# Attention with a complex state and two expert mixtures: plain float32 products in place of three rounded ones

## What is computed

```python
# first mixture; N, D, E, F = 3072, 384, 8, 1024
do_compute = (x @ w_skip) > 0
e_idx = np.argmax(xc @ w_gate, axis=1)            # xc = x[do_compute]
for e in range(E):
    h = np.maximum(xc[mask] @ w1[e], 0.0)         # 384 -> 1024
    y[mask] = gate_w[mask, None] * (h @ w2[e])    # 1024 -> 384
out[do_compute] = xc + y
...
# second mixture: router on normalised rows, no skip, no residual
for e in range(E):
    h = np.maximum(x[mask] @ w1[e], 0.0)
    out[mask] = gate_w[mask, None] * (h @ w2[e])
```

## Time and profile before

| | before |
|---|---|
| median of three runs | 805.1 us |
| profiled execution: its time | 804.9 us |
| profiled execution: its span | 803.0 us |
| mean granted TensorE clock | 0.951 |
| PE, PE weight load busy | 700.5 us, 622.4 us |
| DVE, ACT busy | 657.8 us, 476.1 us |
| POOL busy | 212.9 us |
| first matmul of slot 0 | 372.87 us |
| start of the last matmul of slot 23 | 798.04 us |

### The profile page before, as it was taken

One profiled execution on the slowest core, in us unless ns is written; L12 is line 12 of the kernel. 1 busy time (PEld: TensorE's weight loads), 2 busy tenths in 40 slices (PEclk: granted clock), 3 DMA queues, 4 the chain that ended last, 5 costly groups with the idle time before them and its releaser, 6 DMA issues.

```text
span 803.0 us, 17480 instructions
## 1 busy us (share of the span) xinstructions
PE 700.5 (87%) x6568; PEld 622.4 (78%) x6568; DVE 657.8 (82%) x1241; ACT 476.1 (59%) x660; POOL 212.9 (27%) x184
## 2 busy tenths in 40 slices
PE   0577867169999999947999999999999999999997
PEld 0323332158888888847999998998999999999997
DVE  7998999989999999967888767756898696676672
ACT  7678988566676676552656544646544545544541
POOL 3000000031111111105153566532344322233422
PEclk9888989579999999977999999999999999999999
DMA  7463643017853332455666866776565755756630
GB/s 192 152 216 124 207 161 109 0 34 147 158 145 101 108 118 89 166 116 177 203 220 202 278 222 205 238 222 219 192 216 180 265 192 191 245 208 188 245 139 30
DMA packets 90900, 136.85 MB, mean 170 GB/s; under 512 B 22474, under 2 KB 70070, under 8 KB 90656
## 3 DMA queue, kind: packets, MB, share of 16 engines
q1 hardware_dynamic: 83680, 119.54, 47.9%
q0 software_dynamic: 7168, 16.64, 5.8%
HBM read 124.15 MB, written 14.01 MB: 172 GB/s over the span
## 4 chain that ended last, share of the span: by engine, by line
PE 47%; DVE 4%; DMA 2%; issue 1%; ACT 1%; POOL 0%; POOLq 0%; SPq 0%; DVEq 0%
PE banks L1385 23%; PE banks L1342 22%; PE banks L1328 2%; DVE mix_spot L1578 1%; DVE w_lo L972 1%; DMA raw<-w1b 1%; DMA mix_rows<-xbuf,lists 1%; DVE mix_hT_lo L1677 0%; DMA xbuf<-mix_y,to_scatter 0%; PE banks L1320 0%; ACT mix_hT_hi L1425 0%; DVE mix_y L1701 0%; ACT w_hi L961 0%; POOL to_scatter L1218 0%; POOLq L1091 0%
## 5 line engine op out<-in xcount | busy, mean ns | idle before, releaser
L1342 PE MATMUL banks<-mix_xT_hi,w_hi 128*128 128x240 f32 x576 | 158.8, 276 | 0.6 <-DVE mix_xT_lo L1686 0.6
L1342 PE MATMUL banks<-mix_xT_lo,w_hi 128*128 128x240 f32 x576 | 158.9, 276 | 0.0
L1342 PE MATMUL banks<-mix_xT_hi,w_lo 128*128 128x240 f32 x576 | 158.8, 276 | 0.0
L1385 PE MATMUL banks<-w_hi,mix_hT_hi 128*128 128x384 f32 (+3 forms) x384 | 135.7, 353 | 3.8 <-DVE mix_hT_lo L1677 3.8
L1385 PE MATMUL banks<-w_lo,mix_hT_hi 128*128 128x384 f32 (+3 forms) x384 | 129.8, 338 | 0.0
L1385 PE MATMUL banks<-w_hi,mix_hT_lo 128*128 128x384 f32 (+3 forms) x384 | 129.7, 338 | 0.0
L1425 ACT ACTIVATE mix_hT_hi<-banks 128x480 fp32r<-128x480 f32 x96 | 54.8, 572 | 111.0 <-PE banks L1342 106.0
L1342 PEld LDWEIGHTS banks<-mix_xT_hi,w_hi 128*128 128x128 f32 x576 | 109.5, 190 | 0.9 <-issue 0.8
L1342 PEld LDWEIGHTS banks<-mix_xT_hi,w_lo 128*128 128x128 f32 x576 | 109.6, 190 | 0.0
L1342 PEld LDWEIGHTS banks<-mix_xT_lo,w_hi 128*128 128x128 f32 x576 | 109.5, 190 | 0.0
L1677 DVE SCALAR_TENSOR_TENSOR mix_hT_lo<-banks,mix_hT_hi 128x480 fp32r<-128x480 f32 x96 | 62.7, 653 | 50.5 <-ACT mix_hT_hi L1425 50.4
(11 more groups left out here) (230 smaller groups left out, 1469.0 us busy)
## 6 DMA issues: line engine op xcount, KB each, us to landing
raw<-w1b SPq DMA_DIRECT2D x16, 1536.0 KB, 7.9
raw<-w2b SPq DMA_DIRECT2D x16, 1536.0 KB
A<-w2a_t SPq DMA_DIRECT2D x8, 1536.0 KB, 8.4
raw<-w1a SPq DMA_DIRECT2D x8, 1536.0 KB
raw<-w2a SPq DMA_DIRECT2D x8, 1536.0 KB
ring<-a SPq DMA_DIRECT2D x9, 864.0 KB, 5.1
qk<-q SPq DMA_DIRECT2D x48, 96.0 KB, 2.3
qk<-k SPq DMA_DIRECT2D x48, 96.0 KB, 2.3
```

The source lines that it names most:

```text
L1342: last = pe.matmul(pU[g % TURNS][:, n * N:(n + 1) * N], w1p[m][:, b, c, f * P:(f + 1) * P], xT[s][:, c, 0:N], start=(c == 0 and (s, m) == ...
L1385: last = pe.matmul(pD[0:m, half, 0:ph.width], hT[s][:, f, half * P:half * P + m], w2p[w][:, b, f, 0:ph.width], start=(f == 0 and (s, w) == ...
```

## The change

The mixtures' operands become plain float32 arrays, `xT`, `hT`, `w1` and `w2`, and each product is one `matmul` call on them. All splitting of weights, tokens and hidden numbers goes, on ACT and on DVE; ACT's ReLU (`hidden`) and its copy of the transposed tokens (`copy_x`) write the operands alone. Weights are loaded by DMA straight into the buffers that TensorE reads, two for each layer, by the parity of the slot. They are loaded two slots ahead: `load1(later)` once the first layer of this slot is done (`h_made`), `load2(later)` once its second layer is done (`y_made`). At the start, SP issues the second layer's weights of slot 0 and both layers' weights of slot 1 one after another. The semaphores for loads and scatters come in pairs, one for each parity. The transposes no longer wait for `y_ready`. ACT squares the results of the slot before (`square_y`) one step earlier, and DVE finishes both halves of the slot before ahead of everything else.

```diff
-        self.raw1 = raw1
-        self.raw2 = sbuf("raw2", [P, FC, DM + E])
-        self.hi1, self.lo1 = (sbuf(f"w1_{part}", [P, 2, KC, F], F32R) for part in ("hi", "lo"))
-        self.hi2, self.lo2 = (sbuf(f"w2_{part}", [P, 2, FC, DM + E], F32R) for part in ("hi", "lo"))
+        self.w1 = (raw1, sbuf("w1_odd", [P, KC, F]))
+        self.w2 = tuple(sbuf(f"w2_{b}", [P, FC, DM + E]) for b in range(2))
...
+    def load1(self, sp, slot, e):
+        w1 = slot.ph.weights[0][bass.ds(e, 1)].rearrange("e (c p) f -> p (e c) f", p=P)
+        sp.dma_start(self.w1[slot.b][:, :, :], w1).then_inc(slot.ph.loaded1[slot.b], 16)
...
-            weights.load(sp, Slot(phases[0], 0, 0, 0, 0), None, 0)
+            weights.load2(sp, Slot(phases[0], 0, 0, 0, 0), 0)
+            weights.load1(sp, Slot(phases[0], 0, 1, 1, 1), 1)
+            weights.load2(sp, Slot(phases[0], 0, 1, 1, 1), 1)
...
+                    sp.wait_ge(ph.h_made, slot.j * NG + NG)
+                    sp.sem_inc(weights.carrier, 1)
+                    weights.load1(sp, later, e)
...
+                if later is not None:
+                    sp.wait_ge(ph.y_made, slot.j * SUB + SUB)
+                    sp.sem_inc(weights.carrier, 1)
+                    weights.load2(sp, later, e)
...
-                pe.wait_ge(ph.lo1_ready, slot.j * 2 + 2)
-                pe.wait_ge(ph.x_lo, slot.j * SUB + SUB)
+                pe.wait_ge(ph.loaded1[b], slot.i * 16 + 16)
+                pe.wait_ge(ph.x_ready, slot.j * SUB + SUB)
...
-                            for s, m in PASSES:
-                                last = pe.matmul(pU[g % TURNS][:, n * N:(n + 1) * N],
-                                                 w1p[m][:, b, c, f * P:(f + 1) * P], xT[s][:, c, 0:N],
-                                                 start=(c == 0 and (s, m) == PASSES[0]),
-                                                 stop=(c == KC - 1 and (s, m) == PASSES[-1]))
+                            last = pe.matmul(pU[g % TURNS][:, n * N:(n + 1) * N],
+                                             weights.w1[b][:, c, f * P:(f + 1) * P], xT[:, c, 0:N],
+                                             start=(c == 0), stop=(c == KC - 1))
...
-                        for s, w in PASSES:
-                            last = pe.matmul(pD[0:m, half, 0:ph.width], hT[s][:, f, half * P:half * P + m],
-                                             w2p[w][:, b, f, 0:ph.width],
-                                             start=(f == 0 and (s, w) == PASSES[0]),
-                                             stop=(f == FC - 1 and (s, w) == PASSES[-1]))
+                        last = pe.matmul(pD[0:m, half, 0:ph.width], hT[:, f, half * P:half * P + m],
+                                         weights.w2[b][:, f, 0:ph.width], start=(f == 0), stop=(f == FC - 1))
...
                 hidden(slot, 0)
-                if nxt is not None and (ph.n, slot.at) != (0, 0):
-                    weights.hi_part1(act, nxt, 0)
-                hidden(slot, 1)
-                if nxt is not None and (ph.n, slot.at) != (0, 0):
-                    weights.hi_part1(act, nxt, 1)
```

More of the change, by code:

```diff
@@ L951, in part @@
[L951 to L974, removed]
@@ L984, with load2 @@
+    def load2(self, sp, slot, e):
+        ph, into = slot.ph, self.w2[slot.b]
+        w2 = ph.weights[1][bass.ds(e, 1)].rearrange("e (c p) f -> p (e c) f", p=P)
+        sp.dma_start(into[:, :, 0:w2.shape[2]], w2).then_inc(ph.loaded2[slot.b], 16)
+        if ph.scored:
+            sp.dma_start(into[:, :, w2.shape[2]:], ph.scoring[bass.ds(e, 1)].rearrange("e p c k -> p (e c) k")
+                         ).then_inc(ph.loaded2[slot.b], 16)
 class Phase:
@@ L1197, in body @@
                                  ).then_inc(routing_loaded, 16)
+                if later is not None:
+                    sp.wait_ge(ph.y_made, slot.j * SUB + SUB)
+                    sp.sem_inc(weights.carrier, 1)
+                    weights.load2(sp, later, e)
             tail, _ = stream(sp, phases, E, body)
             for ph in phases:
-                for s in range(SUB):
-                    sp.wait_ge(ph.scattered[s], tail.j * 16 + 16 if ph is tail.ph else 16 * E)
+                for done in ph.scattered[0] + ph.scattered[1]:
+                    sp.wait_ge(done, tail.i * 16 + 16 if ph is tail.ph else 8 * E)
                     sp.sem_inc(weights.carrier, 1)
@@ L1350, in body @@
                     pe.wait_ge(weighed, 2 if slot.at == 0 else 3)
-                pe.wait_ge(ph.lo2_ready, slot.j * 2 + 2)
+                pe.wait_ge(ph.loaded2[b], (slot.i * 16 + 16) * (2 if ph.scored else 1))
                 by_token(slot, before, nxt)
@@ L1391, in by_token @@
                         if (half, f) in TURNS_AT and nxt is not None:
-                            turn_next(before, nxt, half)
+                            turn_next(nxt, half)
                         if half == 0:
@@ L1705, in body @@
                 at = (ph.n, slot.at)
-                hidden(slot, 0)
                 if before is not None:
-                    finish(before, oldest, 0)
-                hidden(slot, 1)
-                if before is not None:
-                    finish(before, oldest, 1)
+                    for s in range(SUB):
+                        finish(before, oldest, s)
                 if at == (0, "close0"):
@@ L1715, in body @@
                     spots(phases[2])
-                if nxt is not None and at != (0, 0):
-                    weights.lo_part1(dve, nxt, 0)
-                hidden(slot, 2)
-                if nxt is not None and at != (0, 0):
-                    weights.lo_part1(dve, nxt, 1)
-                hidden(slot, 3)
                 if at == (1, 7):
                     over_entries(phases[2])
-                if at == (0, 0):
-                    weights.lo_part1(dve, nxt, 0)
-                    weights.lo_part1(dve, nxt, 1)
                 if at == (0, 0):
```

126 lines of the change are left out of this document (30 added, 96 removed).

## The result

The change makes the kernel slower: 886.75 us (median of four runs, 885.36 to 886.85) against 804.2 us (four runs, 801.23 to 806.18), a ratio of 1.1029 with a 95% interval of 1.0996 to 1.1063. The forecast was 889 us. In the changed kernel the first layer is line L1305, the second L1344, the transposes of tokens L1292.

The account below looks back on a forecast made before the run. The prediction took PE's matmuls, end to end in the mixtures, to bound the kernel. Products +86.5, waits -3.8 and start +1.6 us gave +84.3 us on 804.9, so 889 us, range 880 to 905.

Parts of the forecast that it names:

- The step that carries the prediction: Mixtures' matmuls on PE: two instructions a call, two cycles a column plus 3 ns each; +86.5 us over 24 slots.
- The step of -3.8 us: Second layer: PE's six waits for the hidden numbers' low part go and nothing replaces them; -3.8 us.
- Loads: Weight loads in the slots: issued about 30 us ahead of use, longest load 9.5 us, so costed at nothing.
- The +1.6 us: Before slot 0: second half's gather lands 2.2 us later behind added loads, less 0.6 us; bounds -0.6 to +5.3 us.
- The 0.6 us of DVE's split: Before slot 0: DVE's split of the tokens goes, so up to 0.6 us comes back.
- The forecast's sum: Whole kernel: products +86.5, waits -3.8 and start +1.6 us make +84.3 us.
- The rival in which the float32r extra stays with plain products: Both layers: each plain instruction has 9 and 13 ns more than taken; +20 us, 910 us; chance 0.07.
- four passes at today's price: Both layers: each call costs four of today's matmuls, not three; +5.5 us a slot, 935 us in all; chance 0.03.
- The faster rival: Mixtures: a call is one stream at two cycles a column, weight loads bind at 15.8 us a slot; 771 us; chance 0.03.

Follow-up runs that it names:

- cols256: The changed kernel with the first 128 output columns of the second layer left out: 803.31 us in a single run.
- the two one-layer kernels: The kernel before with plain float32 in the first layer alone, 837.03 us, or in the second layer alone, 846.42 us, against 803.91 us.
- calm: The kernel before with only order changed (DVE's spots after the low parts, routing table loaded one slot later): 799.22 us against 804.73.
- half_calls: The changed kernel without every second block of hidden numbers in both layers in phases 1 and 2: 724.21 us in a single run.
- late_loads: The changed kernel with slot 1's loads issued only after slot 0's tokens have landed: 884.18 us, ratio 1.0986 to the kernel before.
- the two in bfloat16: The kernel before with bfloat16 high and low parts, 779.25 us against 804.73, and the same with reordered spots and routing table load, 769.69 us against 804.04.
- the bfloat16 kernel: The kernel before with bfloat16 in place of float32r for the high and low parts: 779.25 us against 804.73, ratio 0.9689.

## Why the prediction was right, point by point

**Products.** The step that carries the prediction held to 0.02 us a slot: 9.74 us was the forecast for the first layer and 9.72 is measured, 10.34 + 0.63 for the second and 10.98, 10.55 + 0.63 in phase 0 and 11.19. The sum over the slots is 16 x 3.57 + 8 x 3.64 = 86.2 us, forecast 86.5. Two instructions for a call and two cycles for a column, read from the plain products of the first stages, hold in the mixtures. `cols256` shows the column rate by itself, the two one-layer kernels show that the loss is the sum of the layers. The Trainium skill's half rate for FP32_LOW_HIGH (Perfetto Trace Analysis, Engine Utilization) agrees with the trace if it is read as that of one instruction: 0.3225 us for 384 columns. For the whole product the Trainium skill's four passes (FP8 and Floating Point Precision, TensorE Precision Notes) agree with it, two instructions of two cycles a column each.

**Waits.** The step of -3.8 us was mis-sized, as it took the idle column for the price: `calm` measures 5.3 us for the same waits. The mechanism was right, and as forecast nothing replaced them.

**Loads.** Costed at nothing, and PE never waited for a weight. `half_calls` shows the cover to be larger than I argued.

**Start.** The +1.6 us had the right place but the wrong gather. The first half's gather was late, by 1.1 us; the second half's, forecast 2.2 us late, landed 3.4 us after its issue, where the kernel before had its transposes 4.1 us after. The 0.6 us of DVE's split didn't come back as a whole either: ACT's copy ended at 372.91, and slot 0 began only behind the filler at the half clock, 0.38 us later, for 0.69 in the kernel before. Slot 0 began at 373.29 for 372.87, +0.4 us, and slot 0 itself lost less to the half clock than in the kernel before: it is 0.80 us longer than slot 1 there, against 1.77. Together -0.5 us in this pair of profiles. This part varies with where the clock rises: in six profiles of kernels with the same filler (before, changed, `late_loads`, `calm`, the two in bfloat16) it first came up between 366.6 and 375.6 us, so from these profiles the start can be foretold to about 2 us only. The forecast had the half clock in slot 0 stay or grow, and it shrank from 3.3 us to 1.6. That the start lies just within its bounds (-0.6 to +5.3 us) is in part luck.

**The sum.** 86.2 - 5.3 - 0.5 = 80.4 us; the two spans differ by 883.1 - 803.0 = 80.1. The forecast's sum was 84.3: 2.1 us of the difference lie in the start, 1.5 in the waits, 0.3 in the slots. The medians differ by 82.55, as the profiled execution was the fastest of the changed kernel's four, 1.4 us below their median, and that of the kernel before 0.7 us above its own. The rival in which the float32r extra stays with plain products fell with the 0.2025 us of the first layer, and four passes at today's price with it.

**The faster rival** was never near, but its arithmetic was wrong: `half_calls` has about the work of PE that one instruction for a call would leave, and its slots are PE's 10.68 us and not 15.8.

## What to carry to other kernels

Before replacing a split product by a plain one, count the instructions and the cycles a column of a plain product elsewhere in the same trace, and multiply: four cycles for three lost here, where TensorE has no gaps, although DVE was rid of 239 us and ACT of 132. What DVE and ACT save is worth only the waits that name them, and a wait's price is read from distances of starts, not from the idle column. Where TensorE binds, look at the distance from one start to the next against the stream's columns: 12 to 16 ns over it on each of 2880 matmuls, for 2.5 to 3 with another type of coarser parts, were 1.29 us a slot here, 31 us in all.

## What the runs showed of the hardware

- Matmuls with float32r operands follow each other in 0.112 us with 240 columns and 0.176 with 384; with bfloat16 in 0.1025 and 0.163; plain float32 in 0.2025 and 0.3225, twice one cycle a column and 2.5 ns. The type alone makes the products of a slot 8% cheaper (15.2 us for 16.5).
- In the bfloat16 kernel PE stood for 2.8 us from 481.9 on, waiting for DVE's low part, after work almost without a gap, and the clock fell to the half level (1.2 GHz) from 484.4 to 487.8. The windows, columns as above:

```profile
481.00:484.40 3.40, 0.90 (x16) 0.48 (x14) 3.40 (x4) 0.44 (x1) 3.11 (x1) 1.00 0.03 5
484.40:487.80 3.40, 3.11 (x17) 1.90 (x18) 2.47 (x3) 0.13 (x1) 2.50 (x2) 0.50 0.14 19
```

- The same filler ahead of slot 0 had the full clock in the kernel before from 366.6 us on (it fell again at 373.5, in slot 0), and the half clock in the changed kernel up to 374.9. Why it rose in one and not in the other isn't shown. The windows, the kernel before first:

```profile
366.60:373.40 6.80, 3.82 (x48) 3.02 (x47) 6.23 (x10) 0.92 (x2) 5.58 (x5) 1.00 0.38 92
...
366.60:373.40 6.80, 4.85 (x42) 4.59 (x42) 3.96 (x15) 0.92 (x2) 5.28 (x5) 0.50 0.67 172
```
